# Attention and two gated layers on one core: scores of the fifth query tile by the whole array, and a new nominal timetable

## The chip, the cores and the metric

The kernel runs on one core of a Trainium2 chip. The core has five engines that run at their own pace and meet at semaphores: PE (TensorE, matrix products, with weight loads shown as PEld), DVE (VectorE), ACT (ScalarE), POOL (GpSimd) and SP (SyncE, which here only issues transfers). The metric is the time of one execution on the device in microseconds (us). Before the change the median of three runs is 757.01 us (756.95 to 757.7).

## The reference

Three stages follow each other. All inputs and outputs are float32.

```
scores = (q @ k.T) / sqrt(64)              # 4 batches, 8 heads, 576 positions, head width 64
mask   = (i // 64) >= (j // 64)            # block i sees blocks 0..i
attn   = exp(scores - max) / (sum + 1e-9);  x = attn @ v          # 2304 tokens x 512

h      = x @ w_in                          # 512 -> 1024
solu   = h * softmax(h);  ln = (solu - mean) / sqrt(var + 1e-6) * g_ln
x2     = ln @ w_out                        # 1024 -> 512

h      = x2 @ w_in2                        # 512 -> 2048
g      = h * tanh(softplus(h));  out = g @ w_out2                 # 2048 -> 512
```

## The kernel before, in words

**Precision.** Each float32 operand of a product is kept as a high float16 half and a low one (what is left after rounding). A product is three matmuls added in one bank: high by high, low by high, high by low. The halves are made by ACT (high) and DVE or POOL (low).

**Attention.** The 576 positions of a batch are cut in five query tiles: four of 128 queries (two blocks of 64) and a fifth of 64 queries (one block). Heads go in pairs, the first head of a pair in partitions 0 to 63, the second in 64 to 127. A unit `u` is one batch, one tile and one pair of heads: 80 units, numbered 20 to a batch, so units 16 to 19 of a batch are its fifth tile. For each unit PE computes scores (`score`, L704), DVE takes the row maximum (L883), ACT the exponential (L1035), DVE the reciprocal of the sum (L889), POOL multiplies by it (`normalise`, L618), PE transposes in rounds of up to four 128x128 blocks (`turn`, L718), ACT and DVE split what comes out (`high` L1045, `low` L895), and PE multiplies by v (`values`, L743). In `score` the two heads are two matmuls on quarters of the array, 64 rows by 64 columns each, which lie on a diagonal and run at the same time. For the fifth tile that is 12 matmuls a unit: three terms by two heads over 512 keys, and again over the last 64.

**Queries.** A tile of queries for all four pairs is loaded to `q_raw` (two buffers, `load_q`), rounded by ACT to `q_hi` (`q_high`, L1026), and POOL subtracts (`q_low`, L625); only the very first tile is subtracted by DVE. `q_hi` and `q_lo` have two buffers, so tile `a` waits until the scores of tile `a - 2` are done.

**The layers.** Tokens go in nine groups of 256 (two tiles of 128). Per group PE does `solu_in` (L767), four transposes at a time of the normalised tile (`turn_ln`, L780), `solu_out` (L791), `mish_in` (L810) and `mish_out` (L829). Between `solu_in` and `turn_ln` lies a chain of small steps: the maximum (`h1_max`, DVE L927 and L930), the exponential (ACT), `weigh` (DVE L936), squares (ACT), `variance` (DVE L943 to L947), `root` (ACT) and `norm_ln` (DVE L954 to L958). Weights come in 24 pieces; ACT and DVE split 20 of them (`w_high`, `w_low` L915), POOL the last four (`w2_split`, L649 to L653). `solu_out` of the first group may start only when the low halves of pieces 4 and 5 are there.

**What sets the order.** Every step has a nominal time in the table `TIMES`, in units of 10 ns. `PLAN` is all 2146 steps sorted by it, and every engine takes its own steps out of `PLAN` in that order. The times set only the order; what an engine waits for is fixed by semaphores. So a step that stands early on an in-order engine holds back all that follows it there.

## Time and profile before

| | |
|---|---|
| median of three runs | 757.01 us (756.95 to 757.7) |
| the profiled execution, whole | 755.96 us |
| its span, first to last instruction | 754.2 us |
| PE busy | 730.6 us, 97% of the span |
| DVE, ACT, POOL busy | 365.4, 367.0 and 158.2 us |
| granted clock of PE | full, but for one stretch of 6.8 us from 46.1 us |
| last matmul group ends | 751.1 us, followed by one copy and one store |

A line of the timeline gives the start, the duration, the engine, the line of the kernel, what is written from what, the part of the array (rows times columns), the size of the moving operand, and how many instructions were merged. Matmuls are pipelined: each lasts longer than the distance to the next one, so the pace is read from starts, not from durations.

### The profile page before, as it was taken

Reading aid. Unit: us, or ns where it says so; the run is one execution under the profiler, and the core shown is the slowest. Engines: PE = TensorE matmul, PEld = TensorE weight load, DVE = VectorE, ACT = ScalarE, POOL = GpSimd, SP = SyncE. Lnnn points to the kernel's source line nnn. Section 1 sums busy time; section 2 is a strip of 40 time slices with the busy share of each in tenths; the row PEclk is TensorE's granted clock in tenths of the full one; section 3 lists DMA queues with packets and bytes.
Section 4 is the critical chain, followed back from the end, with each engine's and each line's share of the span. In section 5 each row is a group of like instructions: output and inputs, shape, how many; then the busy total and the mean of one; then the engine's idle time right before and its main releaser. Section 6 shows DMA issues by size and latency. Waiting matters only on the chain.

```text
span 754.2 us, 16392 instructions
## 1 busy us (share of the span) xinstructions
PE 730.6 (97%) x6880; PEld 502.4 (67%) x6880; DVE 365.4 (48%) x777; ACT 367.0 (49%) x822; POOL 158.2 (21%) x257
## 2 busy tenths in 40 slices
PE   4879999999999999999999999999999999999998
PEld 3448955677577856685578657774678567856773
DVE  4898888433752456324633375335533553243120
ACT  4878854355534454354535554464444543443140
POOL 4542356520111022220211013411110111000000
PEclk9989999999999999999999999999999999999999
DMA  8337331200000011020000001110000000000000
GB/s 298 119 96 251 105 100 63 92 8 16 15 2 29 11 36 48 19 95 2 1 29 16 15 1 61 33 36 1 2 16 2 15 1 16 2 15 15 1 15 28
DMA packets 16120, 32.50 MB, mean 43 GB/s; under 512 B 1968, under 2 KB 5552, under 8 KB 16048
## 3 DMA queue, kind: packets, MB, share of 16 engines
q1 hardware_dynamic: 16048, 31.47, 12.7%
q8 instruction: 54, 0.88, 0.5%
q14 instruction: 18, 0.15, 0.1%
HBM read 26.74 MB, written 4.72 MB: 42 GB/s over the span
## 4 chain that ended last, share of the span: by engine, by line
PE 92%; DVE 5%; ACT 1%; issue 1%; DMA 1%; POOL 0%; SPq 0%; ACTq 0%; DVEq 0%
PE banks L810 25%; PE banks L829 24%; PE banks L791 13%; PE banks L767 11%; PE banks L718 6%; PE banks L704 6%; PE banks L743 5%; PE banks L780 2%; DVE pT_lo L895 1%; DMA solu<-va 1%; DVE stat L927 1%; DVE solu L936 0%; ACT prob L1035 0%; DVE k_hi L857 0%; ACT pT_hi L1045 0%
## 5 line engine op out<-in xcount | busy, mean ns | idle before, releaser
L810 PE MATMUL banks<-x2T_hi,WH 128*128 128x256 f16 x576 | 157.1, 273 | 0.0
L810 PE MATMUL banks<-x2T_lo,WH 128*128 128x256 f16 x576 | 157.0, 273 | 0.0
L810 PE MATMUL banks<-x2T_hi,WL 128*128 128x256 f16 x576 | 157.0, 273 | 0.0
L618 POOL TENSOR_SCALAR prob<-prob,rinv 128x64 f32<-128x64 f32 (+8 forms) x144 | 77.5, 550 | 344.9 <-DVE rinv L889 344.9
L1045 ACT ACTIVATE pT_hi<-banks 128x512 f16<-128x512 f32 (+2 forms) x128 | 64.3, 502 | 133.4 <-PE banks L718 113.2
L895 DVE TENSOR_TENSOR pT_lo<-banks,pT_hi 128x512 f16<-128x512 f32 (+2 forms) x128 | 72.9, 570 | 103.4 <-ACT pT_hi L1045 102.7
L829 PE MATMUL banks<-WH,gT_hi 128*128 128x512 f16 x288 | 109.3, 380 | 0.0
L829 PE MATMUL banks<-WH,gT_lo 128*128 128x512 f16 x288 | 109.2, 379 | 0.0
L829 PE MATMUL banks<-WL,gT_hi 128*128 128x512 f16 x288 | 109.2, 379 | 0.0
L1035 ACT ACTIVATE prob<-banks,nmax 128x64 f32<-128x64 f32 (+8 forms) x144 | 74.9, 525 | 57.6 <-DVE nmax L883 34.1
L980 DVE SCALAR_TENSOR_TENSOR gT_lo<-gbuf,gT_hi 128x512 f16<-128x512 f32 x72 | 52.1, 731 | 103.6 <-ACT gT_hi L1118 103.4
L1111 ACT ACTIVATE gbuf<-banks 128x512 f32<-128x512 f32 x72 | 42.8, 596 | 89.1 <-PE banks L810 83.9
L883 DVE TENSOR_REDUCE nmax<-banks 128x1 f32<-128x64 f32 (+8 forms) x144 | 64.0, 482 | 37.1 <-PE banks L704 37.0
L791 PE MATMUL banks<-lnT_hi,WH 128*128 128x256 f16 x288 | 78.6, 273 | 0.0
L791 PE MATMUL banks<-lnT_hi,WL 128*128 128x256 f16 x288 | 78.5, 273 | 0.0
L791 PE MATMUL banks<-lnT_lo,WH 128*128 128x256 f16 x288 | 78.5, 273 | 0.0
L718 PE MATMUL banks<-ident,prob 128*128 128x128 f32 x400 | 68.6, 283 | 3.0 <-DVE pT_lo L895 2.2
L810 PEld LDWEIGHTS banks<-x2T_hi,WH 128*128 128x128 f16 x576 | 56.3, 98 | 9.5 <-issue 0.6
L810 PEld LDWEIGHTS banks<-x2T_lo,WH 128*128 128x128 f16 x576 | 56.4, 98 | 8.4
L810 PEld LDWEIGHTS banks<-x2T_hi,WL 128*128 128x128 f16 x576 | 56.4, 98 | 6.5
L718 PEld LDWEIGHTS banks<-ident,prob 128*128 128x128 f32 x400 | 46.8, 142 | 17.4 <-issue 4.9
L767 PE MATMUL banks<-WH,xTh 128*128 128x512 f16 (+1 forms) x160 | 54.8, 380 | 0.7 <-DVE xTl L903 0.7
(90 smaller groups left out, 1217.9 us busy)
## 6 DMA issues: line engine op xcount, KB each, us to landing
w_raw<-w SPq DMA_DIRECT2D x12, 512.0 KB, 5.1
out<-osb SPq DMA_DIRECT2D x18, 256.0 KB, 2.0
q_raw<-q SPq DMA_DIRECT2D x16, 256.0 KB, 3.0
k_raw<-k SPq DMA_DIRECT2D x12, 288.0 KB, 3.4
v_raw<-va SPq DMA_DIRECT2D x12, 256.0 KB, 2.6
ln_raw<-w SPq DMA_DIRECT2D x6, 512.0 KB, 3.9
own_raw<-w SPq DMA_DIRECT2D x4, 512.0 KB, 3.7
solu<-w SPq DMA_DIRECT2D x2, 512.0 KB, 4.1
```

The source lines that it names most:

```text
L618: pool.tensor_scalar(of, of, rinv[:, u % 2, i:i + 1], S_X, ALU.mult, ALU.mult).then_inc(norm_done, 1)
L704: mm = pe.matmul(scores[BLOCK * c:BLOCK * (c + 1), at + lo:at + last], qq[rows, z, queries(tile) * p + n * i:queries(tile) * p + n * (i + 1)],
L718: mm = pe.transpose(banks[:, t_bank(n), P * at:P * (at + 1)], prob[:, u % 2, 512 * i + P * c:512 * i + P * (c + 1)], ident[:])
L767: mm = pe.matmul(h1_of(t)[lo:hi, half], (xTh, xTl)[a][:, c, col:col + hi - lo], w1i(b, c, half), start=(c == 0 and i == 0), stop=(c == DMC ...
L791: mm = pe.matmul(banks[:, X2_BANK[c // 2], G * (c % 2):G * (c % 2 + 1)], w1o(b, j, c), (lnT_hi, lnT_lo)[a][:, j], start=(c % 2 == 0 and j ...
L810: mm = pe.matmul(banks[:, MI_BANK[n % 2], G * j:G * (j + 1)], w2i(b, c, m), (x2T_hi, x2T_lo)[a][:, c], start=(c == 0 and i == 0), stop=(c ...
L829: mm = pe.matmul(banks[:, MO_BANK[i]], (gT_hi, gT_lo)[a][:, m, P * i:P * (i + 1)], w2o(b, m), start=(m == 0 and term == 0), stop=(m == F2C ...
L883: dve.tensor_reduce(nmax[:, u % 2, i:i + 1], scores[:, at:at + width(blk)], AX_X, ALU.max, negate=True).then_inc(max_done, 1)
L895: dve.tensor_tensor(pT_lo[:, u % 2, 4 * rnd:4 * rnd + size].rearrange("r a n -> r (a n)"), banks[:, t_bank(n), 0:P * size], pT_hi[:, u % 2 ...
L980: dve.scalar_tensor_tensor(out=gT_lo[:, 2 * n:2 * n + 2].rearrange("r c n -> r (c n)"), in0=gbuf[:, n % 2], scalar=S_G, in1=gT_hi[:, 2 * n ...
L1035: act.activation(prob[:, u % 2, 512 * i:512 * i + width(blk)], scores[:, at:at + width(blk)], ACT.Exp, bias=nmax[:, u % 2, i:i + 1], scale ...
L1045: act.activation(pT_hi[:, u % 2, 4 * rnd:4 * rnd + size].rearrange("r a n -> r (a n)"), banks[:, t_bank(n), 0:P * size], ACT.Copy).then_in ...
```

## The change

Two things are changed together.

The queries of the fifth tile get buffers of their own, `d_hi` and `d_lo`. For each pair they hold 128 columns: the first head's 64 queries in partitions 0 to 63 and columns 0 to 63, the second head's in partitions 64 to 127 and columns 64 to 127, and zeros elsewhere, written once by DVE at the start. With these as weights one matmul on the whole array gives the scores of both heads, so that a unit of the fifth tile has six matmuls. Each half of the queries is now a separate ACT instruction and a separate DVE instruction (`q_low_fifth`); POOL no longer takes part in these four tiles. They wait for the scores of the previous batch's fifth tile only.

The nominal times of all steps are new, and with them the order on every engine.

```
--- before.py
+++ after.py
@@ -99,6 +99,11 @@
+def q_parts(a):
+    return a + 1 + (a + 1) // 5
@@ -210,179 +215,179 @@
 TIMES = {
-    "score": (620, 647, 908, 1046, 1427, 1470, 1727, 1772, 2440, 2943, 3366, 3830, 4729, 5404, 5732, 6756, 9438,
+    "score": (620, 652, 908, 954, 1387, 1491, 1848, 1922, 2411, 3011, 3433, 3786, 4349, 5045, 5864, 6607, 7367, 9576,
...
@@ -415,6 +420,8 @@
         k_raw = sb("k_raw", [P, 2, SEQ], F32)
         v_raw = sb("v_raw", [P, 2, KCH, P], F32)
         q_hi, q_lo = sb("q_hi", [P, 2, PAIRS * P], F16), sb("q_lo", [P, 2, PAIRS * P], F16)
+
+        d_hi, d_lo = sb("d_hi", [P, PAIRS, 2, BLOCK], F16), sb("d_lo", [P, PAIRS, 2, BLOCK], F16)
         k_hi, k_lo = sb("k_hi", [P, PAIRS, SEQ], F16), sb("k_lo", [P, PAIRS, SEQ], F16)
         v_hi, v_lo = sb("v_hi", [P, PAIRS, KCH, P], F16), sb("v_lo", [P, PAIRS, KCH, P], F16)
         prob = sb("prob", [P, 2, 1024], F32)
@@ -445,6 +452,7 @@
         g_in, g_scaled = sem("g_in"), sem("g_scaled")
         const_pool, const_dve = sem("const_pool"), sem("const_dve")
         q_hi_done, q_lo_done = sem("q_hi_done"), sem("q_lo_done")
+        d_lo_done = sem("d_lo_done")
         k_hi_done, k_lo_done = sem("k_hi_done"), sem("k_lo_done")
         v_hi_done, v_lo_done = sem("v_hi_done"), sem("v_lo_done")
         w_hi_done, w_lo_done = sem("w_hi_done"), sem("w_lo_done")
@@ -534,13 +542,21 @@
             token = P * tile + P - 1
             return 5 * (token // SEQ) + token % SEQ // P + 1
 
+        def wait_queries(eng, a):
+
+            if a % 5 == 4:
+                eng.wait_ge(d_lo_done, 2 * (a // 5 + 1))
+            else:
+                eng.wait_ge(q_lo_done, a + 1 - a // 5)
+
         @block.sync
         def _(sp):
 
             def load_q(a):
                 b, tile = a // 5, a % 5
                 n = PAIRS * queries(tile)
-                wait(sp, q_lo_done, a - 1)
+                if a >= 2:
+                    wait_queries(sp, a - 2)
                 sp.dma_start(q_raw[:, a % 2, 0:n], q[b, :, 512 * tile:512 * tile + n]).then_inc(q_in[a % 2], 16)
 
             def load_k(n):
@@ -621,7 +637,7 @@
             def q_low(a):
                 z, n = a % 2, PAIRS * queries(a % 5)
                 wait(pool, s_done, subs(4 * (a - 1)) if a > 1 else 0)
-                pool.wait_ge(q_hi_done, a + 1)
+                pool.wait_ge(q_hi_done, q_parts(a))
                 pool.tensor_tensor(q_lo[:, z, 0:n], q_raw[:, z, 0:n], q_hi[:, z, 0:n], ALU.subtract).then_inc(q_lo_done, 1)
 
             def v_halves(hi, lo, raw, n):
@@ -667,7 +683,7 @@
                     v_split(*of)
                 if kind == "norm":
                     normalise(*of)
-                if kind == "q_low":
+                if kind == "q_low" and of[0] % 5 < 4:
                     q_low(*of)
                 if kind == "w2_split":
                     w2_split(*of)
@@ -680,31 +696,35 @@
                 z = u // 4 % 2
                 blocks = blocks_of(tile)
                 if p == 0:
-                    pe.wait_ge(q_lo_done, u // 4 + 1)
+                    wait_queries(pe, u // 4)
                 if b == 0 and tile == 0:
                     pe.wait_ge(k_lo_done, p // 2 + 1)
                 elif tile == (0 if b else 2):
                     pe.wait_ge(k_lo_done, keys_split(4 * b + p))
                 by_block = in_quarters(u) and in_quarters(u - 1)
-                n = queries(tile) // len(blocks)
                 for i in range(len(blocks)):
                     if by_block:
                         pe.wait_ge(exp_done, subs(u - 1) + i + 1)
                     elif i == 0:
                         wait(pe, exp_done, subs(u - 1 if u < EARLY else u) if u else 0)
+                if tile == 4:
+                    for lo, hi in ((0, 512), (512, SEQ)):
+                        for term, (qq, kk) in enumerate(((d_hi, k_hi), (d_lo, k_hi), (d_hi, k_lo))):
+                            mm = pe.matmul(scores[:, lo:hi], qq[:, p].rearrange("r h n -> r (h n)"), kk[:, p, lo:hi],
+                                           start=(term == 0), stop=(term == 2))
+                    mm.then_inc(s_done, 1)
+                    return
 
                 for group in ([range(len(blocks))] if in_quarters(u) else [[i] for i in range(len(blocks))]):
-                    for lo, hi in [(0, 512)] + [(512, SEQ)] * (tile == 4):
-                        for term, (qq, kk) in enumerate(((q_hi, k_hi), (q_lo, k_hi), (q_hi, k_lo))):
-                            for i in group:
-                                last = min(width(blocks[i]), hi)
-                                for h in range(2):
-                                    rows, c = slice(DH * h, DH * (h + 1)), row_half(u, i, h)
-                                    at = s_place(u, i)
-                                    mm = pe.matmul(scores[BLOCK * c:BLOCK * (c + 1), at + lo:at + last],
-                                                   qq[rows, z, queries(tile) * p + n * i:queries(tile) * p + n * (i + 1)],
-                                                   kk[rows, p, lo:last], start=(term == 0), stop=(term == 2),
-                                                   skip_group_check=True)
+                    for term, (qq, kk) in enumerate(((q_hi, k_hi), (q_lo, k_hi), (q_hi, k_lo))):
+                        for i in group:
+                            for h in range(2):
+                                rows, c = slice(DH * h, DH * (h + 1)), row_half(u, i, h)
+                                at = s_place(u, i)
+                                mm = pe.matmul(scores[BLOCK * c:BLOCK * (c + 1), at:at + width(blocks[i])],
+                                               qq[rows, z, P * p + BLOCK * i:P * p + BLOCK * (i + 1)],
+                                               kk[rows, p, 0:width(blocks[i])], start=(term == 0), stop=(term == 2),
+                                               skip_group_check=True)
                 mm.then_inc(s_done, len(blocks))
 
             def turn(u, rnd):
@@ -863,6 +883,14 @@
                 dve.wait_ge(q_hi_done, 1)
                 dve.tensor_tensor(q_lo[:, 0], q_raw[:, 0], q_hi[:, 0], ALU.subtract).then_inc(q_lo_done, 1)
 
+            def q_low_fifth(a):
+                wait(dve, s_done, subs(4 * (a - 4)) if a > 4 else 0)
+                raw = q_raw[:, a % 2, 0:PAIRS * BLOCK].rearrange("r (p n) -> r p n", p=PAIRS)
+                for h in range(2):
+                    rows = slice(DH * h, DH * (h + 1))
+                    dve.wait_ge(q_hi_done, q_parts(a) - 1 + h)
+                    dve.tensor_tensor(d_lo[rows, :, h], raw[rows], d_hi[rows, :, h], ALU.subtract).then_inc(d_lo_done, 1)
+
             def k_first(j):
                 pairs = slice(2 * j, 2 * j + 2)
                 dve.wait_ge(k_first_in[j], 16)
@@ -982,7 +1010,11 @@
                                          op0=ALU.mult, op1=ALU.subtract).then_inc(g_lo, 1)
 
             dve.memset(v_raw[64:P, :, 4], 0.0).then_inc(const_dve, 1)
+            dve.memset(d_hi[:], 0.0).then_inc(const_dve, 1)
+            dve.memset(d_lo[:], 0.0).then_inc(const_dve, 1)
             for kind, *of in PLAN:
+                if kind == "q_low" and of[0] % 5 == 4:
+                    q_low_fifth(*of)
                 if kind == "q_first":
                     q_first()
                 if kind == "k_first":
@@ -1022,8 +1054,16 @@
             def q_high(a):
                 z, n = a % 2, PAIRS * queries(a % 5)
                 act.wait_ge(q_in[z], 16 * (a // 2 + 1))
-                wait(act, s_done, subs(4 * (a - 1)) if a > 1 else 0)
-                act.activation(q_hi[:, z, 0:n], q_raw[:, z, 0:n], ACT.Copy).then_inc(q_hi_done, 1)
+                if a % 5 == 4:
+                    wait(act, s_done, subs(4 * (a - 4)) if a > 4 else 0)
+                    act.wait_ge(const_dve, 3)
+                    raw = q_raw[:, z, 0:n].rearrange("r (p n) -> r p n", p=PAIRS)
+                    for h in range(2):
+                        rows = slice(DH * h, DH * (h + 1))
+                        act.activation(d_hi[rows, :, h], raw[rows], ACT.Copy).then_inc(q_hi_done, 1)
+                else:
+                    wait(act, s_done, subs(4 * (a - 1)) if a > 1 else 0)
+                    act.activation(q_hi[:, z, 0:n], q_raw[:, z, 0:n], ACT.Copy).then_inc(q_hi_done, 1)
 
             def exps(u, i):
                 b, tile, p = place(u)
```

The order on PE, at the first score of a fifth tile, before:

```order
L704 MATMUL banks<-k_hi,q_hi 64x512 x2
L704 MATMUL banks<-k_hi,q_lo 64x512 x2
L704 MATMUL banks<-k_lo,q_hi 64x512 x2
L704 MATMUL banks<-k_hi,q_hi 64x64 x2
L704 MATMUL banks<-k_hi,q_lo 64x64 x2
L704 MATMUL banks<-k_lo,q_hi 64x64 x2
L743 MATMUL banks<-pT_hi,v_hi 64x128 x2
```

and after:

```order
L713 MATMUL banks<-k_hi,d_hi 128x512
L713 MATMUL banks<-k_hi,d_lo 128x512
L713 MATMUL banks<-k_lo,d_hi 128x512
L713 MATMUL banks<-k_hi,d_hi 128x64
L713 MATMUL banks<-k_hi,d_lo 128x64
L713 MATMUL banks<-k_lo,d_hi 128x64
L830 MATMUL banks<-x2T_hi,WH 128x256
```

The twelve matmuls on quarters of the array have become six on the whole of it; the products that follow differ too, since the place of the score moved.

The order on DVE in the first group of tokens, before. `stat` and `solu` belong to the layers' chain, `WL` is the low half of a piece of weights, `pT_lo` and `nmax` belong to attention. L958 at the end is the normalisation of the first tile:

```order
L915 SCALAR_TENSOR_TENSOR WL<-own_raw,gsc,WH 128x512 x2
L943 TENSOR_SCALAR stat<-stat 128x1
L944 SCALAR_TENSOR_TENSOR stat<-stat 128x1
L947 SCALAR_TENSOR_TENSOR stat<-stat 128x1
L895 TENSOR_TENSOR pT_lo<-banks,pT_hi 128x512
L927 TENSOR_REDUCE stat<-banks 128x1
L930 TENSOR_SCALAR stat<-stat 128x1
L915 SCALAR_TENSOR_TENSOR WL<-w_raw,gsc,WH 128x512 x2
L954 SCALAR_TENSOR_TENSOR stat<-stat 128x1
L956 TENSOR_SCALAR stat<-stat 128x1
L957 TENSOR_SCALAR stat<-stat 128x1
L958 TENSOR_SCALAR solu<-solu,stat 128x1024
```

and after, around the normalisation of the second tile, where the lines are 28 higher (L958 is L986, L915 is L943):

```order
L971 TENSOR_SCALAR stat<-stat 128x1
L972 SCALAR_TENSOR_TENSOR stat<-stat 128x1
L975 SCALAR_TENSOR_TENSOR stat<-stat 128x1
L911 TENSOR_REDUCE nmax<-banks 128x1 x2
L982 SCALAR_TENSOR_TENSOR stat<-stat 128x1
L984 TENSOR_SCALAR stat<-stat 128x1
L985 TENSOR_SCALAR stat<-stat 128x1
L986 TENSOR_SCALAR solu<-solu,stat 128x1024
L923 TENSOR_TENSOR pT_lo<-banks,pT_hi 128x256
L943 SCALAR_TENSOR_TENSOR WL<-own_raw,gsc,WH 128x512 x2
L994 TENSOR_TENSOR lnT_lo<-banks,lnT_hi 128x4x128
L943 SCALAR_TENSOR_TENSOR WL<-w_raw,gsc,WH 128x512 x2
```

Pieces 4 and 5 of the weights (two instructions each) stood ahead of the first tile's normalisation; now they stand behind the second tile's, with the split of a transposed bank between them.

The order on DVE in the second group, behind the normalisation of its first tile, before:

```order
L958 TENSOR_SCALAR solu<-solu,stat 128x1024
L889 RECIPROCAL rinv<-rsum 128x1
L857 TENSOR_SCALAR k_hi<-k_raw 128x576
L859 SCALAR_TENSOR_TENSOR k_lo<-k_raw,k_hi 128x576
L936 ISA solu,stat<-banks,solu 128x1024
L936 ISA stat 128x1
```

and after:

```order
L986 TENSOR_SCALAR solu<-solu,stat 128x1024
L964 ISA solu,stat<-banks,solu 128x1024
L964 ISA stat 128x1
L966 TENSOR_SCALAR stat<-stat 128x1
L923 TENSOR_TENSOR pT_lo<-banks,pT_hi 128x128
L994 TENSOR_TENSOR lnT_lo<-banks,lnT_hi 128x4x128
```

The split of a pair's keys (L857, L859) stood between the normalisation and the next tile's `weigh` (L936); in the new order it stands behind the second tile's chain, and `weigh` comes at once.

## Rows read from the trace of the kernel before

**Rows 1.** The page, busy time and share of the span, engine by engine.
```profile
PE 730.6 (97%) x6880; PEld 502.4 (67%) x6880; DVE 365.4 (48%) x777; ACT 367.0 (49%) x822; POOL 158.2 (21%) x257
```

**Rows 2.** Busy time by stretch; columns as the first line says, all in us.
```profile
core 0: us, PE busy (x) PEld busy (x) DVE busy (x) ACT busy (x) POOL busy (x), PEclk, DMA share, GB/s
0.00:80.00 80.00, 62.15 (x668) 42.97 (x669) 63.95 (x137) 58.19 (x136) 30.99 (x61) 0.96 0.57 191
112.00:136.00 24.00, 21.40 (x262) 12.26 (x261) 19.85 (x42) 11.61 (x35) 18.09 (x20) 1.00 0.18 60
160.00:754.20 594.20, 591.05 (x5410) 406.41 (x5408) 246.62 (x542) 267.73 (x590) 86.64 (x151) 1.00 0.06 19
46.10:52.90 6.80, 5.40 (x38) 3.27 (x40) 6.26 (x19) 4.91 (x13) 4.97 (x8) 0.50 0.36 114
```

**Rows 3.** Timeline of PE around one score of a fifth tile: start, us, what.
```profile
97.37 0.27 PE L810 MATMUL banks<-x2T_hi,WL 128*128 128x256 f16 x1
97.57 0.40 PE L704 MATMUL banks<-k_hi,q_hi 64*64 64x512 f16 x2
...
98.25 0.19 PE L704 MATMUL banks<-k_hi,q_hi 64*64 64x64 f16 x2
...
98.43 0.25 PE L743 MATMUL banks<-pT_hi,v_hi 128*64 128x128 f16 x2
```

**Rows 4.** The chain of waits near the end: start, us, what.
```profile
714.67 14.41 PE banks L810 x132
...
734.28 16.85 PE banks L829 x78
```

**Rows 5.** Timeline of PE: values of a fifth tile, two units, then a transpose.
```profile
131.15 0.22 PE L743 MATMUL banks<-pT_hi,v_hi 128*64 128x64 f16 x2
...
132.09 0.20 PE L743 MATMUL banks<-pT_lo,v_hi 128*64 128x64 f16 x2
132.22 0.44 PE L718 MATMUL banks<-ident,prob 128*128 128x128 f32 x2
```

**Rows 6.** Timeline of PE, the longest idle time in the middle of the ramp.
```profile
46.51 1.12 PE L780 MATMUL banks<-ident,solu 128*128 128x128 f32 x4 [3.62 <-DVE solu L958]
```

**Rows 7.** Timeline of DVE in the ramp: start, us, what.
```profile
30.70 0.32 DVE L857 TENSOR_SCALAR k_hi<-k_raw 128x320 f16<-128x320 f32 x1
31.06 0.49 DVE L859 SCALAR_TENSOR_TENSOR k_lo<-k_raw,k_hi 128x320 f16<-128x320 f32 x1
...
39.77 1.41 DVE L915 SCALAR_TENSOR_TENSOR WL<-own_raw,gsc,WH 128x512 f16<-128x512 f32 x2
...
43.63 1.40 DVE L915 SCALAR_TENSOR_TENSOR WL<-w_raw,gsc,WH 128x512 f16<-128x512 f32 x2
...
52.80 0.81 DVE L958 TENSOR_SCALAR solu<-solu,stat 128x1024 f32<-128x1024 f32 x1
...
54.37 1.21 DVE L883 TENSOR_REDUCE nmax<-banks 128x1 f32<-128x448 f32 x2
55.50 0.68 DVE L966 TENSOR_TENSOR lnT_lo<-banks,lnT_hi 128x512 f16<-128x512 f32 x1
```

**Rows 8.** Waits of PE from 112 to 136 us: who for whom, us, times, longest.
```profile
PE banks L718 <- DVE pT_lo L895: 1.7, 1, 1.7
```

**Rows 9.** Timeline of DVE and POOL in the same stretch.
```profile
118.82 2.45 POOL L653 TENSOR_TENSOR WL<-ln_raw,WH 128x1024 f16<-128x1024 f32 x1
119.27 2.31 DVE L857 TENSOR_SCALAR k_hi<-k_raw 128x576 f16<-128x576 f32 x1
...
135.36 0.45 DVE L857 TENSOR_SCALAR k_hi<-k_raw 128x576 f16<-128x576 f32 x1
```

**Rows 10.** Timeline of DVE, its second instruction.
```profile
3.62 0.43 DVE L857 TENSOR_SCALAR k_hi<-solu 128x512 f16<-128x512 f32 x1 [2.50 <-DMA solu<-k]
```

**Rows 11.** Groups of instructions by line and shape: busy us, mean ns, idle before.
```profile
L625 POOL TENSOR_TENSOR q_lo<-q_raw,q_hi 128x256 f16<-128x256 f32 x4 | 2.7, 672 | 5.2 <-ACT q_hi L1026 5.2
...
L1026 ACT ACTIVATE q_hi<-q_raw 128x256 f16<-128x256 f32 x4 | 1.6, 408 | 0.0
```

More of the change, by code:

```diff
@@ new lines @@
+    "norm": (930, 1010, 1214, 1412, 1856, 2008, 2364, 2603, 2919, 3609, 3885, 4596, 5401, 5871, 7280, 8058, 9844,
[5 rows of a table added]
+    "pad": (157, 209, 1809, 2107, 2549, 3316, 4714, 6009, 8336, 9828, 13225, 13581, 14305, 14855, 16042, 17134,
+        20324, 20923, 24158, 25423, 28898, 29608, 30931, 31070, 35983, 36965, 38853, 38869, 42870, 43062, 45181,
+        46438, 47631, 50020, 52109, 52578, 56062, 56912, 60408, 61354),
+    "turn": (985, 1046, 1365, 1582, 1987, 2195, 2474, 2699, 3074, 3496, 3848, 4078, 4262, 4474, 4892, 5346, 5630,
[8 rows of a table added]
@@ new lines @@
+    "high": (1274, 1351, 1604, 1707, 2158, 2295, 2511, 2727, 3309, 3549, 3742, 4132, 4251, 4695, 5017, 5390, 5723,
[8 rows of a table added]
+    "low": (1318, 1394, 1688, 1753, 2239, 2362, 2668, 2904, 3392, 3682, 4004, 4215, 4400, 4835, 5202, 5447, 5856,
[8 rows of a table added]
+    "value": (1556, 1652, 1736, 1831, 2369, 2657, 2891, 2978, 3945, 4936, 4995, 5804, 6685, 6768, 9650, 9726, 12249,
[5 rows of a table added]
+    "x_high": (1870, 3033, 6131, 9815, 13764, 15034, 17604, 21366, 25736, 29674, 32877, 37129, 41017, 43661, 47811,
+        49504, 53328, 57210, 61534, 65308),
@@ new lines @@
+    "load_v": (3200, 4166, 5783, 7712, 12675, 13110, 15394, 14760, 28594, 30302, 30622, 30936, 46036, 47820),
+    "k_split": (1801, 2729, 2808, 3453, 7463, 12314, 12640, 13340, 25680, 26646, 27465, 29051, 44228, 44615, 45052,
+        45273),
+    "v_split": (3038, 4003, 4161, 4438, 12325, 12796, 13610, 14522, 28277, 28665, 30383, 30697, 45276, 46006, 46985,
+        47848),
+    "g_scale": (1723,),
+    "load_w": (1176, 1961, 3296, 2917, 5018, 5295, 5687, 5879, 6633, 6681, 5343, 5200, 7071, 8325, 6585, 8980, 9351,
+        9833, 10380),
@@ new lines @@
+    "weigh": (3249, 4249, 10227, 11120, 18157, 18865, 26359, 27254, 34014, 34955, 42169, 43230, 50095, 50864, 57894,
+        58634, 65872, 66569),
+    "squares": (3407, 4426, 10633, 10919, 18141, 19028, 26486, 27618, 34305, 34786, 42810, 43111, 50315, 50848,
+        58113, 58904, 66091, 66408),
+    "variance": (3533, 4522, 10816, 11719, 18388, 19111, 26509, 28154, 34488, 35788, 42898, 43434, 50302, 51007,
+        58324, 59197, 66259, 66711),
+    "root": (3602, 4591, 10885, 11788, 18460, 19180, 26662, 28223, 34752, 35856, 43019, 43921, 50463, 51612, 58439,
+        59581, 66374, 66872),
@@ L386 @@
+    "copy_out": (12376, 15917, 20169, 25095, 30186, 33051, 37910, 40597, 45872, 48355, 51735, 56490, 61729, 64837,
+        67642, 70381, 72159, 72918),
 }
```

108 lines of the change are left out of this document (40 added, 68 removed), and 204 rows, old and new, of the table TIMES.

## The prediction

> **What bounds the kernel now.** I read the page first. PE is busy 730.6 us of 754.2 while DVE and ACT stand at about half and POOL at a fifth [rows 1], so the time is PE's work plus PE's gaps. Next I looked at where the gaps are, by stretches [rows 2]. From 0 to 80 us PE is idle 80.00 - 62.15 = 17.85 us, from 112 to 136 us 2.6 us, and from 160 us to the end 594.20 - 591.05 = 3.15 us, which is about the last copy and store. In between there is nothing to gain but matmul time itself. The reader should see two regimes: a ramp of 80 us, in which other engines decide, and 670 us in which the only coins are the columns that PE streams and what it loses at joints. Third came the timeline of PE, by distances between starts. At full clock 128x512 matmuls follow each other every 16.85 / 78 = 0.216 us and 128x256 ones every 14.41 / 132 = 0.109 us [rows 4].
>
> **Scores of the fifth tile.** One unit takes 98.43 - 97.57 = 0.86 us [rows 3]; there are 16, all alike. Of that, the three 512-column pairs take 98.25 - 97.57 = 0.68 us and the three 64-column pairs, with the way out, 0.18 us. After: three 128x512 matmuls at 0.216 make 0.648 us, and three with 64 columns on the whole array. The trace has no such matmul. The nearest row from below is the values of a fifth tile, 30 pairs from 131.15 to 132.09 us, or 0.94 / 29 = 0.032 us a pair with 2 x 64 weight columns loaded each time [rows 5]. From above it is the 0.11 us between 128x256 matmuls, which also load 128x128 weights each time [rows 4]; they stream four times the columns. I take 0.04, near the lower end, because the row that moves 64 columns is the closer one. The unit is then 0.77 us, and 16 x (0.86 - 0.77) = -1.4 us. The bounds are 0.744 and 0.978 us a unit: -1.9 to +1.9 us.
>
> The Trainium skill, "TensorE: Matmul & The Clock Gate", section "LDWEIGHTS (loading the stationary operand)", gives columns / 1.2 ns for a weight load: 107 ns for 128 columns, 53 for 64. That speaks against this change, since all weight loads become twice as wide; by it the unit would be 0.648 + 0.32 = 0.97 us. The trace is on neither side for 128 columns, but for 64 the pace of 0.032 us [rows 5] is faster than 53 ns.
>
> **Joints.** Between a matmul on the whole array and one on halves or quarters of it there is a loss. Into a score: 97.57 - 97.37 = 0.20 us where 0.11 would do, so 0.09 [rows 3, 4]. Out of the values into a transpose: 132.22 - 132.09 = 0.13 where 0.03 would do, so 0.10 [rows 5]. Between values and scores I take 0.09 too. In the order of before I count 82 steps on the whole array followed by scores or values, 29 exits from values to the whole array and 15 values followed by scores: 82 x 0.09 + 29 x 0.10 + 15 x 0.09 = 11.6 us. Exits from scores lie in the units' own time. After, with the fifth tile's scores on the whole array and the new order, I count 72, 34 and 9: 6.5 + 3.4 + 0.8 = 10.7 us. That is -0.9 us; between none and the loss going fully, 0 to -1.5.
>
> The Trainium skill, "TensorEngine Tiling (Array Packing)", section "Key Properties", says that changing the tiling mode drains the engine. That is what the 0.09 shows, and the page has no price for it.
>
> **Ramp.** PE's longest gap here is 3.62 us before the transposes of the first tile, and it ends with DVE's normalisation [rows 6]. DVE is the in-order engine whose list decides. On its way from the first maximum of the layers to the second tile's normalisation the new order leaves out both weight pieces, 1.41 + 1.40 us, and the key split of a pair, 0.32 + 0.49, which now goes earlier, and takes in two row maxima of 1.21 us [rows 7]: -2.4 us. But the pieces must come before the first output product. Before, the normalisation ended at 53.61, the last bank needed was split at 56.18 (55.50 + 0.68) and products followed, 2.6 us later [rows 7]. In the new order, behind the normalisation, come a low half of 256 columns, put at 0.4 (below the 0.68 of 512), piece 4 with 1.41, the bank's 0.68 and piece 5 with 1.40, some 3.9 us: +1.3. Net -1.1 us. Moreover one more score of an eighth block, 0.77 us of PE work, now stands ahead of that product, in time that PE would wait. Sum -1.9; I take -1.8. PE works at half clock from 46.1 to 52.9 us, 5.4 us of it busy [rows 2]; at full clock this work would take 2.7 us less. Just before it fell from 2.4 to 1.2 GHz the engine had been idle for most of the 3.62 us that end at 46.51 [rows 6]. The new order breaks that idle time in smaller parts, but I see others of the same sum, so I leave the clock as it is and keep 2.7 us as a bound on both sides. Bounds of the ramp: -4.5 and +2.7 us.
>
> **The second group, 112 to 136 us.** The largest of PE's waits is 1.7 us for the low half of a transposed block [rows 8]. DVE was late because a key split stood between the normalisation and `weigh`: it took 2.31 us, against 0.45 for the same instruction later, while POOL subtracted a weight piece from 118.82 to 121.27 [rows 9]. In the new order this split stands behind the second tile's chain. I expect 1.2 of the 2.6 us idle back; bounds 0 and -2.6.
>
> The Trainium skill, "SBUF — State Buffer", section "Who interferes with whom", says that DVE in a two-port mode and GpSimd hold it in turn for a whole instruction. This trace agrees: 119.27 + 2.31 is 0.3 us after POOL's end. It means that the new order can meet the same collision elsewhere.
>
> **The rest.** The two zero fills on DVE stand at the start, where DVE idles 2.50 us until the first keys land [rows 10]; free, and POOL waits for the fill before them only. POOL loses 4 x 0.67 us of subtraction and gives it to DVE [rows 11], as eight instructions of at most 0.49 us each, the price of the 320-column low half [rows 7]; ACT has eight instructions in place of four of 0.41 us [rows 11]. DVE and ACT are at half load, so these are covered after 160 us; without cover they would cost 3.9 us and 1.6 us at most in all. `load_q` waits for the same events in substance. From 160 us to the end PE has no waits to give back; I take -0.2 us for small ones.
>
> **Sum.** -1.4 - 0.9 - 1.8 - 1.2 - 0.2 = -5.5 us. The profiled execution took 755.96 us; it becomes 750.5. The median of the runs shown lies 1.05 us above the profiled execution, so the median after should be 751.5 us.
>
> **Rivals.** (1) The weight loads bound the short matmuls: 0.11 us for each of the three, the unit 0.978 in place of 0.77 us, so +3.3 us on the sum, 754.8. For it: no row shows 128 weight columns loaded faster than every 0.11 us. Against: the pace of the values.
> (2) The order gives nothing in the ramp and in the second group, because another step takes the place of the one that was late, such as ACT's exponential or a transfer: only the scores and joints remain, -2.5 us, 754.5.
> (3) Slower: the two weight pieces behind the second normalisation are not absorbed. It decides if that normalisation comes no earlier than before: then the first output product waits for both, +2.8 us, PE's idle time grows to a second half-clock stretch, +2.7, and with the scores, joints and the rest at -2.5 and nothing from the second group, 757.0 + 3.0 = 760.0. DVE has 63.95 us of work in the first 80 [rows 2], which speaks for it; the 2.4 us taken out ahead speak against.
> (4) The change does not do what it says: the twelve matmuls ran two at a time already, so six of them stream the same 1728 columns. Then the unit costs 0.86 still, and only order and joints count, 752.9.
>
> **How the numbers follow.** My forecast, with all terms of that sign, has 0.60; (1) 0.10, (2) 0.13, (3) 0.10, (4) 0.07. A difference below 0.2% (1.5 us) can't be told from none here. Faster than 755.5: the forecast nearly whole, (4), and most of (1) and (2), 0.80. Within 755.5 to 758.5: their edges and a mild (3), 0.10. Slower: 0.10. The range goes from 747.5, where the ramp's clock stretch goes too, to 756.5, which takes in (1) and (2) and leaves (3) out.
>
> **What would show it.** In the changed profile, a fifth-tile score should take about 0.77 us from its first matmul to the next step's, with no 0.09 us joint before it after a whole-array step; the 64-column starts lie 0.03 to 0.05 us apart (right) or 0.11 (rival 1). The first output product should start before 55.5 us, against 56.2 or later. PE's idle time should fall to about 16 us in the first 80 us and below 1.5 in the second group. After 160 us the idle time should stay at about 3 us; anything above says that the new order waits somewhere. A half-clock stretch longer than 7 us would make me wrong on the slow side, and none at all would make me too careful.

## The result and the profile after

| | before | after |
|---|---|---|
| median of 4 runs, us | 756.98 (755.41 to 757.7) | 748.75 (748.3 to 749.24) |
| profiled execution, us | 755.96 | 749.24 |
| its span, us | 754.2 | 747.1 |
| PE idle, 0 to 80 us | 17.85 | 18.23 |
| PE idle, 112 to 136 us | 2.60 | 0.00 |
| PE idle, 160 us to the end | 3.15 | 3.09 |

The ratio is 0.9894 (95%: 0.9877 to 0.9911), a gain of 8.2 us at the medians and of 6.7 us between the two profiled executions, whose spans differ by 7.1 us. Forecast were 5.5.

The page of the kernel after, busy time by engine, to be read against [rows 1]:

```profile
PE 725.8 (97%) x6784; PEld 501.7 (67%) x6784; DVE 365.1 (49%) x787; ACT 369.4 (49%) x826; POOL 158.4 (21%) x253
```

PE has 96 matmuls fewer. DVE and ACT have 10 and 4 instructions more, and their work has hardly changed. The stretches of the kernel after, which answer to [rows 2]; the last two are those at half clock:

```profile
core 0: us, PE busy (x) PEld busy (x) DVE busy (x) ACT busy (x) POOL busy (x), PEclk, DMA share, GB/s
0.00:80.00 80.00, 61.77 (x666) 43.00 (x667) 63.30 (x137) 55.98 (x133) 32.58 (x59) 0.96 0.55 187
112.00:136.00 24.00, 24.00 (x217) 15.46 (x216) 16.62 (x40) 10.64 (x29) 14.05 (x13) 1.00 0.14 39
160.00:747.10 587.10, 584.01 (x5322) 402.83 (x5319) 250.62 (x546) 268.48 (x590) 84.42 (x145) 1.00 0.06 20
46.00:49.40 3.40, 3.40 (x22) 1.77 (x20) 2.87 (x8) 2.32 (x4) 2.51 (x4) 0.50 0.04 11
52.80:56.20 3.40, 3.40 (x49) 2.71 (x51) 3.40 (x6) 1.32 (x3) 0.00 (x0) 0.50 0.42 105
```

Two surprises stand here. The ramp has not become shorter for PE, and in the second group no idle time is left. The half-clock time is still 6.8 us in sum, but it now comes as two stretches in which PE is busy throughout.

The timeline of PE around a fifth-tile score of the kernel after (start, us, what) answers to [rows 3]:

```profile
78.79 0.27 PE L830 MATMUL banks<-x2T_hi,WL 128*128 128x256 f16 x1
78.90 0.38 PE L713 MATMUL banks<-k_hi,d_hi 128*128 128x512 f16 x1
...
79.55 0.19 PE L713 MATMUL banks<-k_hi,d_hi 128*128 128x64 f16 x1
79.58 0.19 PE L713 MATMUL banks<-k_hi,d_lo 128*128 128x64 f16 x1
...
79.64 0.27 PE L830 MATMUL banks<-x2T_hi,WH 128*128 128x256 f16 x1
```

From 78.90 to 79.64 are 0.74 us, against 0.86 before. The short matmuls start 0.03 us apart, and in front of the unit stands only the 0.11 us of a 256-column matmul: the joint is gone.

PE in the ramp of the kernel after (in brackets its idle time before the row, and what ended it):

```profile
42.27 0.60 PE L800 MATMUL banks<-ident,solu 128*128 128x128 f32 x4
...
45.73 0.88 PE L738 MATMUL banks<-ident,prob 128*128 128x128 f32 x4 [1.44 <-DVE pT_lo L923]
...
52.19 0.66 PE L800 MATMUL banks<-ident,solu 128*128 128x128 f32 x4 [2.68 <-DVE solu L986]
...
53.56 0.32 PE L763 MATMUL banks<-pT_hi,v_hi 128*64 128x128 f16 x2
53.67 0.31 PE L763 MATMUL banks<-pT_hi,v_lo 128*64 128x128 f16 x2
...
55.62 0.64 PE L724 MATMUL banks<-k_hi,q_hi 64*64 64x448 f16 x4
...
56.65 0.66 PE L800 MATMUL banks<-ident,solu 128*128 128x128 f32 x4
57.15 0.27 PE L811 MATMUL banks<-lnT_hi,WH 128*128 128x256 f16 x1
```

The first output product of the kernel before, from its own timeline:

```profile
56.27 0.27 PE L791 MATMUL banks<-lnT_hi,WH 128*128 128x256 f16 x1
```

The first tile's transposes start at 42.27 us, 4.2 us before those of [rows 6]; the first output product at 57.15, against 56.27 before. In between PE waits 2.68 us for the second tile's normalisation. Then eighteen value pairs, 0.056 us each at full clock, go at 0.107 us. The score that now stands ahead of this product takes 1.03 us from its first matmul to the next step (55.62 to 56.65), the first part of it at half clock.

DVE there, which answers to [rows 7]:

```profile
51.32 0.81 DVE L986 TENSOR_SCALAR solu<-solu,stat 128x1024 f32<-128x1024 f32 x1
...
52.38 1.41 DVE L943 SCALAR_TENSOR_TENSOR WL<-own_raw,gsc,WH 128x512 f16<-128x512 f32 x2
...
54.30 1.40 DVE L943 SCALAR_TENSOR_TENSOR WL<-w_raw,gsc,WH 128x512 f16<-128x512 f32 x2
```

The normalisation (L986) comes at 51.32 instead of 52.80 us. The two weight pieces end at 55.70, ahead of PE: DVE is not the last wait before the product any more, PE's own queue at half clock is.

DVE in the second group of the kernel after, against [rows 9]:

```profile
115.26 1.19 DVE L986 TENSOR_SCALAR solu<-solu,stat 128x1024 f32<-128x1024 f32 x1
116.38 1.21 DVE L964 CUSTOM_DVE_ANT_0 solu<-banks,solu 128x1024 f32<-128x1024 f32 x1
```

The next tile's first step (L964) follows the normalisation at once; before, the key split stood between them.

**Where the time went.** I took the start of the last output product in both profiled executions and subtracted from it all PE work ahead of it, each kind at its shortest distance between starts. It moved by 7.1 us. Of that, 2.0 us are the scores, 16 x (0.857 - 0.734), with the starts taken to the nanosecond. The joints are 1.0, by the counts of the prediction (115 in place of 126): 16 fewer into scores and values at 0.093 us, 5 more out of the values at 0.10 us. The remaining 4.2 us are PE's idle and slow time, which falls from 29.0 to 24.8 us (both figures depend by some 0.3 us on what is taken as shortest): some 3.3 in the second group, 1.2 in small pieces after it, and -0.3 in the first 80 us.

### The profile page after: what moved, and what is told of

The parts are those of the page before. It is cut to its first block, busy times and chain, and to the rows that moved or that the text cites. A ratio compares the mean times of both kernels' runs of the same rounds, so it can differ in the third digit from the quotient of the medians.

```text
span 747.1 us, 16209 instructions
## 1 busy us (share of the span) xinstructions
PE 725.8 (97%) x6784; PEld 501.7 (67%) x6784; DVE 365.1 (49%) x787; ACT 369.4 (49%) x826; POOL 158.4 (21%) x253
## 4 chain that ended last, share of the span: by engine, by line
PE 95%; DVE 2%; ACT 1%; DMA 1%; POOL 1%; issue 0%; SPq 0%; ACTq 0%; DVEq 0%
PE banks L830 25%; PE banks L849 25%; PE banks L811 13%; PE banks L787 12%; PE banks L738 6%; PE banks L763 5%; PE banks L724 4%; PE banks L800 2%; PE banks L713 2%; DMA solu<-va 1%; DVE pT_lo L923 0%; DVE nmax L911 0%; POOL prob L634 0%; DVE WL L943 0%; ACT pT_hi L1085 0%
## 5 line engine op out<-in xcount | busy, mean ns | idle before, releaser
L634 POOL TENSOR_SCALAR prob<-prob,rinv 128x64 f32<-128x64 f32 (+8 forms) x144 | 81.2, 575 | 353.6 <-DVE rinv L917 353.6
```

Of the source, the lines that this page charges most:

```text
L634: pool.tensor_scalar(of, of, rinv[:, u % 2, i:i + 1], S_X, ALU.mult, ALU.mult).then_inc(norm_done, 1)
```

## The experiments

All ratios are to the kernel before, run on the same chip; its medians there lay near 756.5 us. Where a difference to the kernel after (748.75 us) is given, it is one between medians, and that kernel's own ratio is known to 1.3 us either way. "Theory" and "rival" are as the expectations name them.

**The two halves of the change.** First the new scores with the nominal times of before, and the new times with the old scores (there, so that no engine waits for ever for a step behind it, the rounding and subtraction of a fifth tile's queries stand behind an exponential wherever the new order had them earlier).

```diff
 # scores_alone: matmuls, query splits and waits of the change; TIMES of before
 # order_alone: TIMES of the change; q_high, q_low and scores of before, and
+for a in (4, 9, 14, 19):
+    last = ("exp", 4 * (a - 1) - 1, len(blocks_of((a - 2) % 5)) - 1)
+    for step in (("q_low", a), ("q_high", a)):
+        if PLAN.index(step) < PLAN.index(last):
+            put(step, last)
```

> The new scores of the fifth tile with the nominal times of before. Theory of the three terms: the unit falls from 0.857 to 0.734 us (16 times, -2.0) and 12 of 82 joints into scores go (-1.1), so -3.1 us, about 754. Rival (all from the order): no change, 757. Rival (POOL's relief counts too, since the fifth tile's low half moved to DVE): more than -3.5 us, with less idle time of PE between 40 and 160 us.

> The scores of before with the new nominal times; the rounding and subtraction of the fifth tile's queries are put later where their old waits need it. Theory: the order is worth what the two parts leave, -4 us, about 753, nearly all of it between 112 and 136 us. Rival (the two parts need each other, since the new buffers let the queries be split early): less than -2 us, with waits of PE for the queries of the fifth tile.

Measured: scores alone 756.76 us, ratio 1.0004 (0.9994 to 1.0014); order alone 752.56, 0.9948 (0.9934 to 0.9962). The second was foreseen; the first gave nothing, although its unit takes 0.734 us in its trace and 12 joints are gone. Its PE waits from 112 to 136 us (who for whom, us, times, longest), windows, and PE's timeline:

```profile
PE banks L738 <- DVE pT_lo L923: 2.1, 1, 2.1
PE banks L800 <- DVE solu L986: 0.8, 1, 0.8
```

```profile
112.00:136.00 24.00, 21.07 (x243) 11.29 (x242) 19.52 (x40) 10.88 (x32) 16.74 (x18) 0.93 0.19 60
126.30:129.70 3.40, 3.40 (x21) 1.26 (x20) 1.34 (x6) 1.39 (x8) 0.78 (x3) 0.51 0.28 87
```

```profile
126.10 0.44 PE L738 MATMUL banks<-ident,prob 128*128 128x128 f32 x1 [2.08 <-DVE pT_lo L923]
126.33 0.63 PE L849 MATMUL banks<-WH,gT_hi 128*128 128x512 f16 x1
126.76 0.63 PE L849 MATMUL banks<-WH,gT_lo 128*128 128x512 f16 x1
```

PE comes earlier, DVE does not, and the wait grows. Behind the wait of 2.08 us the granted clock falls to half, and 512-column matmuls go 0.43 us apart instead of 0.216. Idle and slow time rises by 4.6 us to 33.6 in its profile. Some 1.3 of this are a worse start (its first output product comes at 57.59 us), 1.9 lie in the second group, and 1.5 come behind 160 us, where PE waits at 217 us for 0.4 and at 604 us for 0.5. The last two eat the 3.1 of scores and joints. In the order-alone kernel PE is busy for all 24.00 us of the second group. Its one new wait after 160 us (1.1 us at 207) is for POOL's `normalise`: POOL had idled 7.16 us in front of a query subtraction at 205.69 us that this kernel has to do late.

**The key split in the second group.** Three kernels move it alone: back in the kernel after, later in the kernel before, and later together with the new scores.

```diff
 # keys_back, on the kernel after
+put(("k_split", 5), ("norm_ln", 0, 0))
+put(("k_split", 6), ("k_split", 5))
 # keys_later, on the kernel before; scores_keys_later, on scores_alone
+put(("k_split", 6), ("variance", 0, 1))
```

The kernel before has one key split in that place, keys back has two.

> The changed kernel with the key splits of pairs 5 and 6 put back between the normalisation of the second group's first tile and the next tile's weigh. Theory (this place made DVE late and PE idle): +2.5 to +4 us, about 752, with PE waits of 2 us or more for low halves or the second normalisation from 112 to 136 us. Rival (the gain there came from the order of the PE steps, which now has more layer products between the transposes): within 1 us of the changed kernel, 749.

> The kernel before with one step moved: the key split of pair 6 goes behind the second tile's variance, 6 steps later on DVE. Theory (it held DVE for 3.5 us while PE waited 1.7 us for a low half and 0.8 for the normalisation): -1.5 to -2.5 us, about 755. Rival (the collision with POOL is what costs, and DVE meets it with another step): within 0.7 us of before, 757, and another DVE step of over 2 us between 112 and 125 us.

> The order of before with the new scores, and the key split of pair 6 behind the second tile's variance. Theory (in the kernel with the new scores alone, what PE saved was lost again because DVE was late from 112 to 135 us and the clock then fell for 3.4 us): with DVE no longer late the scores pay, 1.5 to 3 us less than with the later keys alone (754.3), so 751.3 to 752.8. Rival (the new scores themselves bring a cost, on DVE or in the waits for queries, that cancels them in this order): 753.8 to 755.

Measured: keys back 754.28, 0.9973 (0.9963 to 0.9983), 5.5 us over the kernel after; keys later 754.3, 0.9973 (0.9964 to 0.9982), 2.2 us under before; with the new scores 753.3, 0.9956 (0.9943 to 0.9969). DVE and POOL of the keys-back kernel, then PE's longest wait from 112 to 136 us and a window:

```profile
115.33 2.37 DVE L886 TENSOR_SCALAR k_hi<-k_raw 128x576 f16<-128x576 f32 x1
...
118.41 0.45 DVE L886 TENSOR_SCALAR k_hi<-k_raw 128x576 f16<-128x576 f32 x1
```

```profile
114.94 2.44 POOL L678 TENSOR_TENSOR WL<-ln_raw,WH 128x1024 f16<-128x1024 f32 x1
```

```profile
PE banks L747 <- DVE pT_lo L932: 3.7, 1, 3.7
```

```profile
122.50:129.30 6.80, 5.92 (x21) 3.46 (x22) 3.93 (x11) 2.14 (x7) 0.00 (x0) 0.50 0.00 0
```

The key split takes 2.37 us beside POOL's subtraction and ends 0.3 us after it; 0.7 us later the same instruction takes 0.45. The two splits take 4.2 us in all, against 3.5 of the one before, and stand ahead of the step that leads to PE's wait of 3.7 us. Behind that come 5.92 us of work at half clock, some 3 us lost. The 5.5 us are more than the 2.5 to 4 us expected, which left the clock out, and they undo more than the change had done.

Keys later agrees with its theory, and PE's idle time in the second group falls from 2.60 to 0.82 us. Its rival's sign, another DVE step of over 2 us, is there too, but it isn't new. The kernel before and keys later have the same small step of the first tile's `variance` beside a POOL subtraction (113.64 to 115.76 us in the kernel before):

```profile
113.68 2.10 DVE L944 SCALAR_TENSOR_TENSOR stat<-stat 128x1 f32<-128x1 f32 x1
```

```profile
114.82 2.13 DVE L952 SCALAR_TENSOR_TENSOR stat<-stat 128x1 f32<-128x1 f32 x1
```

The same instruction takes 0.16 us at 127.14 us, and 0.42 at 113.25 us of the kernel after, where POOL's subtraction had ended at 112.94. The new order had freed this too, without my having looked for it.

With the new scores on top of the later keys I had expected 1.5 to 3 us and got 1.0 at the medians (3.1 in units and joints). The intervals of the two ratios overlap, so this 1.0 is uncertain. PE waits again, at 212 us for 0.4 and at 599 for 0.5. ACT's timeline at the first of them:

```profile
210.64 0.84 ACT L1072 ACTIVATE d_hi<-q_raw 64x256 f16<-64x256 f32 x2
211.51 0.60 ACT L1148 ACTIVATE lnT_hi<-banks 128x512 f16<-128x512 f32 x1
```

The query split, now two instructions, stands right ahead of a rounding, DVE's low half comes behind that, and PE waits for it. At the second, DVE's two subtractions of queries (0.87 us from 598.68) stand ahead of the low half. This is the cost on ACT and DVE that the prediction took as hidden. It is real in the old order, and the new order hides it: in the kernel after, PE has no such wait after 160 us.

**The scores by pairs of column halves.** The kernel after with each fifth-tile matmul replaced by two on 64 columns of the array each, same queries with the same zero blocks.

```diff
-mm = pe.matmul(scores[:, lo:hi], qq[:, p].rearrange("r h n -> r (h n)"), kk[:, p, lo:hi],
...
+for h in range(2):
+    mm = pe.matmul(scores[BLOCK * h:BLOCK * (h + 1), lo:hi], qq[:, p, h], kk[:, p, lo:hi],
...
```

> The changed kernel, but each fifth-tile score is a pair of matmuls on the two column halves, with the zero halves of the queries kept as weights: 128 rows by 64 columns, twelve matmuls a unit. The columns streamed are the same. Theory (what the whole array saves is the way in and the way out of a divided array): a unit of 0.80 to 0.86 us in place of 0.734, and joints of 0.09 us back in front of it, +2 to +3.3 us, 751 to 752. Rival (the gain is in quarters against halves of the rows): 0.73 to 0.75 us a unit and less than +1 us.

Measured: 752.03, 0.9942 (0.9927 to 0.9956), so +3.3 us, as the theory had it. Its PE timeline:

```profile
77.43 0.27 PE L831 MATMUL banks<-x2T_hi,WL 128*128 128x256 f16 x1
77.64 0.41 PE L714 MATMUL banks<-k_hi,d_hi 128*64 128x512 f16 x2
...
78.37 0.20 PE L714 MATMUL banks<-k_lo,d_hi 128*64 128x64 f16 x2
78.50 0.28 PE L831 MATMUL banks<-x2T_hi,WH 128*128 128x256 f16 x1
```

From 77.64 to 78.50 are 0.86 us, as before the change, and 0.21 us stand in front where 0.11 would do. So all of the gain of a score is that the array isn't divided: 0.12 us in the unit, of which 0.10 are the way out of its last matmul (0.13 here, 0.03 there), and 0.10 ahead of it. The zero blocks cost nothing.

**The two weight pieces in the ramp.** The kernel after with pieces 4 and 5 about where they stood before.

```diff
+put(("w_high", 5), ("exp", 9, 1))
+put(("w_low", 4), ("low", 8, 1))
+put(("w_low", 5), ("w_low", 4))
```

> The changed kernel with the low halves of weight pieces 4 and 5 ahead of the first tile's normalisation on DVE, as before (and the high half of piece 5 early enough on ACT). Theory (the first output product starts when DVE has done the second normalisation and both pieces, in whatever order, so moving them gave the ramp nothing): the first tile's transposes 2.8 us later, the first output product within 1 us of the changed kernel's, in all -0.7 to +1 us, 748 to 750. Rival (the prediction's: pieces behind the normalisation are partly hidden, worth 1.5 us): +1.3 to +2.8 us, 750 to 751.5.

Measured: 752.97, 0.9954 (0.994 to 0.9967): 4.2 us over the kernel after. I was wrong about it, and the rival too small. DVE and the windows of this kernel:

```profile
54.62 0.81 DVE L997 TENSOR_SCALAR solu<-solu,stat 128x1024 f32<-128x1024 f32 x1
```

```profile
44.90:51.80 6.90, 5.55 (x44) 3.71 (x44) 6.17 (x15) 4.66 (x11) 5.33 (x9) 0.53 0.30 103
55.20:58.60 3.40, 3.12 (x32) 2.79 (x34) 1.25 (x3) 0.60 (x1) 0.00 (x0) 0.55 0.00 0
```

The second normalisation comes 3.30 us later (51.32), the first output product 3.34 us later (60.49 for 57.15), and the half-clock time is 10.2 us instead of 6.8. Moving the pieces was therefore worth its price in this order; the ramp would otherwise have been worse than before.

**The clock in the ramp.** Matmuls whose results nobody reads, put where PE has nothing else to do. They go to a bank that is free at that point.

```diff
 # warm_middle: 6 and 12 matmuls of 512 columns, on the kernel after
+put(("warm", "keys", 6), ("turn", 9, 1))
+put(("warm", "keys", 12), ("turn", 10, 1))
 # warm_both: also transposes of the identity, 18 of them first of all
+PLAN.insert(0, ("warm", "ident", 18))
+put(("warm", "ident", 8), ("score", 1))
+put(("warm", "ident", 4), ("score", 3))
+put(("warm", "ident", 4), ("turn", 0, 0))
+put(("warm", "ident", 7), ("turn", 1, 0))
 # before_warm: 12 and 5 matmuls, on the kernel before
+put(("warm", "keys", 12), ("turn", 9, 1))
+put(("warm", "keys", 5), ("turn", 10, 0))
```

> The changed kernel with 6 and 12 matmuls of keys by keys into a bank that nothing reads, in the two longest idle times of PE in the ramp (behind round 1 of units 9 and 10). They add work that is thrown away. Theory (the second half-clock stretch, 52.8 to 56.2 us, falls on real work and costs 1.7 us): with PE kept busy no stretch there, 1 to 2.5 us less than the changed kernel, 746.3 to 747.7. Rival (PE waits for DVE there, so the clock does not matter): 748.5 to 750, or more where the added matmuls delay a transpose.

> As with the idle time filled in the middle, and with 18 transposes of the identity before the first scores and 8, 4, 4 and 7 in the idle times after units 1 and 3 and rounds of units 0 and 1, thrown away too. Theory (PE works at half clock up to 18.7 us, and part of that is on the path): a further 1 to 2 us less. Rival (the first 20 us are set by transfers, DVE and ACT, and the added transposes get in the way): no gain or up to 1 us more than with the middle filled alone.

> The kernel before with 12 and 5 matmuls, thrown away, behind round 1 of unit 9 and round 0 of unit 10, where PE idles 3.6 and 1.5 us. Theory (its half-clock stretch, 46.1 to 52.9 us, mostly lies over time in which PE waits for DVE): no stretch there, but a gain smaller than in the changed kernel (1.9 us), 0.3 to 1.5 us, 755.1 to 756.3. Rival (PE's lateness feeds the chain of DVE as much as in the changed kernel): 1.5 to 2.5 us, 754 to 755.

Measured: 746.89, 0.987 (0.9856 to 0.9884); 745.65, 0.9854 (0.984 to 0.9868); and on the kernel before 754.8, 0.9982 (0.9973 to 0.9992). So 1.9 us, another 1.2, and 1.7 us. In the kernel before, the median lies in the rival's range, not in the theory's: PE's lateness costs there about as much as in the kernel after, though the interval (0.6 to 2.0 us) doesn't decide it. The ramp of the first:

```profile
46.00:57.00 11.00, 9.89 (x110) 6.33 (x108) 10.64 (x27) 7.58 (x18) 3.04 (x6) 1.00 0.21 62
```

```profile
54.83 0.27 PE L821 MATMUL banks<-lnT_hi,WH 128*128 128x256 f16 x1
```

The granted clock stays at its full level of 2.4 GHz, and the first output product starts at 54.83 in place of 57.15 us. With both, it starts at 53.05. The kernel with both beats the two kernels of the comparison: 3.1 us under the kernel after, 11 under before.

Two more kernels tried to get further. One has 16 instead of 7 transposes behind turn(1,0), and 8 behind value(1). The other has besides these 8 instead of 12 matmuls, and two steps on other engines moved.

```diff
 # warm_and_max
+put(("max", 12), ("norm_ln", -1, 1))
+put(("exp", 12, 0), ("high", 10, 1))
```

> As with both idle times filled, but 16 in place of 7 transposes behind unit 1's round and 8 more behind the values of unit 1. Theory (the remaining half-clock stretch, 18.8 to 22.2 us, follows those idle times and covers 1.7 us of lost work): no stretch below full clock after 6 us, another 1 to 1.7 us less, 744 to 744.7. Rival (POOL and DVE set the first 22 us): 745.3 to 746.5.

> As the one with more transposes, and the row maxima of unit 12 behind the second tile's normalisation on DVE (its first exponential behind a rounding on ACT), with 8 in place of 12 matmuls in the idle time before. Theory (the 3 us before the third round of the layers' transposes is DVE's list, 1.21 us of it these maxima): another 0.6 to 1.2 us less than with more transposes alone. Rival (the weight pieces behind it are what the first output product waits for): no gain.

Measured: 745.7, 0.9857 (0.9843 to 0.987), the same as with both; and 748.39, 0.9896 (0.9881 to 0.9912), 2.7 us worse. In the first, the half-clock stretch moved from 19.0 to 22.4 us to 8.6 to 12.0, but PE's second input product of the ramp starts at 32.68 instead of 32.64 us, behind a wait for DVE in both: other engines set it, as the rival had it. In the second, the weight pieces fell behind the maxima, and from the second tile's first output transposes to the product pass 5.8 us instead of 3.7, with 1.14 us of waiting for the last piece. Another 0.9 us is lost before that, in a start with 6.8 us at half clock from 8.5 us on.

## Why the prediction was right, and where it was not

The direction and the range (747.5 to 756.5) held. The sum, -5.5 us, was 2.7 too small at the medians, and errors of opposite sign partly cancel in it: the ramp gave 2.1 us less than forecast, the other four terms 3.8 us more. Another 1.1 us lies between the spans of the two profiled executions and the medians, and belongs to no term. That the sum came this near is partly luck. Of the signs that the prediction named, the spacing of the short matmuls, the missing joint and the idle time after 160 us came true. The first output product (57.15 us instead of before 55.5) and the idle time of the first 80 us (18.23 us instead of about 16) did not.

**Scores of the fifth tile.** Right in mechanism, too careful in size: -2.0 for -1.4 us. The step that failed is the value of 0.04 us for a short matmul on the whole array. Three of them and the way out take 0.09 us, so 0.03 each: the pace that I had called the bound from below, 0.032 us [rows 5], is nearly the price, and I should have taken it. Rival (1) is refuted by this spacing. The Trainium skill, "TensorE: Matmul & The Clock Gate", section "LDWEIGHTS (loading the stationary operand)", gives 107 ns for 128 columns; here such matmuls follow each other every 30 ns, although the trace shows loads of 98 ns each. So by the measurement, loads do not bound this sequence. Rival (4), that the unit costs 0.86 us still, is refuted by the unit.

**Joints.** -1.0 for -0.9 us, right. The price of 0.09 us into the divided array and 0.10 out of it holds in the kernel after.

**Ramp.** Wrong: nothing for -1.8 us. Two steps failed. The first is the list of DVE work. It had the second tile's normalisation 2.4 us earlier and the product 3.9 us behind its end, so 1.1 us earlier in all. The normalisation came 1.5 us earlier (51.32 for 52.80), and from its end at 52.13 to the product pass 5.0 us. DVE is done at 55.70, but PE's own list of value pairs and the score isn't. The second is the clock: PE ran at half clock from 52.8 to 56.2 us with work in it throughout, whereas the stretch before the change was partly spent waiting (5.4 us of work in 6.8). "I leave the clock as it is" was the wrong choice: the first tile's transposes won 3.5 us, net of the work ahead, and gave all of it back by the first output product. The warm-middle kernel shows the size of the clock's part: with it gone the product starts at 54.83, which is before the 55.5 that I had named. Its 1.9 us are most of the 2.1 that the ramp is short of the forecast. Rival (2) was right for the ramp and wrong for the second group. Rival (3) named this mechanism, a second half-clock stretch, but its condition didn't hold, since the normalisation did come earlier, and the pieces were absorbed.

**Second group.** -3.3 for -1.2 us. The key split was the right place, as keys back and keys later show from both sides. I counted the split's time and a part of the idle time only. All 2.6 us of idle time went, and 0.7 us of slow time with them. Keys later alone gives 2.2 us. A candidate for the rest is the small `variance` instruction that took 2.10 us beside POOL and takes 0.42 now; no experiment isolates it.

**The rest.** -1.2 for -0.2 us, spread over the 600 us behind. I can't give it a single cause; the small waits that the new scores bring in the old order are in neither of the two kernels compared, so they don't explain it.

**What the sum could not show.** The halves measured apart are +0.3 (-0.5 to +1.1) and -4.0 (-5.0 to -2.9) us; together -8.2. Adding terms from one trace assumes that time freed on PE stays freed. With the old order it doesn't: scores and joints give 3.1 us, which the wait on DVE, the fall of the clock behind it and two later waits take back. With the new order the same 3.1 us come through. From order alone to the kernel after are 3.8 us, and 2.0 + 1.0 + 1.1 (the wait at 207 us) make 4.1.

**Left open.** How long PE stays at half clock at the start differs between profiled executions, and with it the start by about 1 us. The kernel before and keys later have the same steps in the same order there, but their scores of 256 columns go 0.11 us and 0.21 us apart:

```profile
20.51 0.27 PE L704 MATMUL banks<-k_hi,q_hi 64*64 64x256 f16 x2
20.62 0.27 PE L704 MATMUL banks<-k_hi,q_lo 64*64 64x256 f16 x2
```

```profile
20.91 0.42 PE L712 MATMUL banks<-k_hi,q_hi 64*64 64x256 f16 x2
21.12 0.42 PE L712 MATMUL banks<-k_hi,q_lo 64*64 64x256 f16 x2
```

By the pace, the first reaches full clock at some 18.8 us and the second at some 23.6; no experiment has isolated what draws it. A comparison of two profiles in the ramp carries this much doubt. What the collision of a key split with POOL costs by itself, without the split's own 0.45 us, was not measured.

## What to carry to other kernels

A score that ran on part of the array cost a joint of 0.09 us and a unit longer by 0.12 us. Filling the unused blocks with zeros, so that the whole array is used, cost nothing here, since PE streams the same columns. But time taken out of the engine that bounds the kernel arrives only if the engine that feeds it isn't late by then: look for its longest wait, and put what stands ahead of the late step and isn't needed yet behind it. And after an idle time look at the granted clock of what follows; here cheap matmuls without use in that idle time were worth 1.2 to 1.9 us in three kernels, and still more of them gave nothing in a fourth.

## What was not expected of the hardware

- Matmuls with 128 x 128 fp16 weights and 64 columns start 0.03 us apart on the whole array. On column halves the three pairs and the way out take 0.19 us, from 78.31 to 78.50.
- Going from whole to divided array costs 0.09 us, by 128*64 halves as by quarters; between matmuls on the whole array nothing is lost.
- The half clock lasted 3.4 us behind an idle time of 2.08 us (scores alone) and 6.8 us behind one of 3.7 us (keys back). It wasn't seen behind the 1.72 us of the kernel before, at 125 us.
- A DVE instruction on 128x1 elements took 2.10 us beside a POOL subtraction of 2.12 us, against 0.16 us for the same instruction later.
- Transposes of the identity bring the clock up. The granted clock of the first microseconds reads full in both traces below, and in that of the kernel before, but the spacing tells otherwise; what the table ahead of the prediction says of the clock leaves this start out. PE's first scores of a 128-column block, in the kernel after:

```profile
8.99 0.33 PE L724 MATMUL banks<-k_hi,q_hi 64*64 64x128 f16 x2
9.08 0.34 PE L724 MATMUL banks<-k_hi,q_lo 64*64 64x128 f16 x2
...
```

and in the kernel with both kinds of thrown-away matmuls, behind 18 transposes that took 4.00 us:

```profile
5.89 0.22 PE L739 MATMUL banks<-k_hi,q_hi 64*64 64x128 f16 x2
5.95 0.22 PE L739 MATMUL banks<-k_hi,q_lo 64*64 64x128 f16 x2
...
```

The distances are 0.09 to 0.11 us in the first and 0.05 to 0.06 in the second: 1.2 GHz against 2.4. The 18 transposes themselves start 0.21 us apart to the last, against 0.11 us for such transposes at full clock, so the clock rose right behind them.
